# Delta-rule attention and two feed-forward layers: the inverses' write-out moved behind the next blocks' read, the read-out cut into 64-by-64 products

## The reference

```python
for t in range(S):                       # state: (B, H, 40, 40)
    y[:, :, t] = einsum('bhd,bhde->bhe', rt, state)
    Sa = einsum('bhde,bhe->bhd', state, at)
    state = state * wt[:, :, None, :] - einsum('bhd,bhe->bhde', Sa, bt)
    state = state + einsum('bhd,bhe->bhde', vt, kt)
x = y.transpose(0, 2, 1, 3).reshape(B * S, H * D)
h = x @ w_in;  solu = h * softmax(h);  x = layernorm(solu) * g_ln @ w_out
h = x @ w2_in; out = (max(h, 0) + alpha * min(h, 0)) @ w2_out
```

## Time and profile before

| | us |
|---|---|
| Time before, median of 3 runs | 1008.28 (1002.13 to 1009.63) |
| The profiled execution's own time | 1000.47 |
| Span of its trace | 998.7 |
| Mean granted TensorE clock | 0.966 |
| `solve_u` of step 0, 2, 20 starts at | 61.57, 97.22, 377.77 |
| Start of the last step (23) | 429.22 |

### The profile page before, as it was taken

How to read it: one execution, slowest core, us unless ns; L and a number is a source line. 1 busy time by engine, 2 the same in 40 slices (tenths; PEclk the granted TensorE clock), 3 DMA queues, 4 the chain that set the end, 5 groups by cost and what they waited for, 6 DMA issues and landing times.

```text
span 998.7 us, 31704 instructions
## 1 busy us (share of the span) xinstructions
PE 911.7 (91%) x13408; PEld 860.7 (86%) x13408; DVE 635.8 (64%) x1087; ACT 477.5 (48%) x1011; POOL 252.4 (25%) x452
## 2 busy tenths in 40 slices
PE   3379989998798987888999999999999999999998
PEld 2378888988797986777899999999999999999998
DVE  8957766776576754557756656565757565565644
ACT  3336655565454654436534435353535344443533
POOL 9577655775567621000000000000000000000000
PEclk9689989999999999998999999999999999999999
DMA  5635655557465552243010000000000000000000
GB/s 159 134 80 138 160 117 123 143 139 172 92 149 160 122 112 60 84 145 109 14 27 1 27 11 17 27 0 26 0 26 0 26 0 26 0 26 14 1 14 14
DMA packets 144095, 67.35 MB, mean 67 GB/s; under 512 B 118844, under 2 KB 129980, under 8 KB 143980
## 3 DMA queue, kind: packets, MB, share of 16 engines
q1 hardware_dynamic: 143980, 65.66, 26.5%
HBM read 45.98 MB, written 19.66 MB: 66 GB/s over the span
## 4 chain that ended last, share of the span: by engine, by line
PE 51%; POOL 15%; DMA 12%; DVE 8%; issue 6%; SPq 4%; ACT 3%; POOLq 0%; ACTq 0%; DVEq 0%
POOL s_x L831 6%; PE acc L1116 6%; POOL s_t L829 5%; PE acc L1117 5%; PE acc L1118 5%; DMA l_scr<-lb 5%; PE mid L1116 4%; PE mid L1117 4%; PE mid L1118 4%; PE bank L1116 3%; PE bank L1117 3%; PE bank L1118 3%; DMA s_in<-l_scr 3%; DMA d_scr<-s_x 3%; PE bank L1149 2%
## 5 line engine op out<-in xcount | busy, mean ns | idle before, releaser
L1382 POOL TENSOR_TENSOR stats<-stats 128x1 f32<-128x1 f32 x24 | 13.2, 549 | 552.3 <-DVE stats L1444 552.3
L1469 DVE SCALAR_TENSOR_TENSOR stage<-mid,slopes 128x512 f32<-128x512 f32 x96 | 66.3, 691 | 105.2 <-ACT slopes L1310 105.2
L1306 ACT ACTIVATE stage<-mid 128x512 f32<-128x512 f32 x96 | 57.1, 594 | 158.2 <-PE mid L1187 158.2
L1116 PE MATMUL acc<-wo_h,act_h 128*128 128x320 f32 x384 | 121.4, 316 | 6.7 <-DVE act_l L1396 5.9
L1117 PE MATMUL acc<-wo_h,act_l 128*128 128x320 f32 x384 | 118.4, 308 | 0.0
L1118 PE MATMUL acc<-wo_l,act_h 128*128 128x320 f32 x384 | 117.9, 307 | 0.0
L1116 PE MATMUL mid<-zT_h,w_h 128*128 128x256 f32 x384 | 108.0, 281 | 3.2 <-DVE zT_l L1396 3.2
L1117 PE MATMUL mid<-zT_h,w_l 128*128 128x256 f32 x384 | 107.6, 280 | 0.0
L1118 PE MATMUL mid<-zT_l,w_h 128*128 128x256 f32 x384 | 107.4, 280 | 0.0
L808 POOL TENSOR_TENSOR al<-al,prod 40x512 f32<-40x512 f32 x48 | 74.0, 1541 | 93.1 <-DMA al<-a_features_first 77.6
L1310 ACT ACTIVATE slopes<-stage,minus_alpha 128x256 f32<-128x256 f32 x192 | 87.3, 502 | 3.1
(11 more groups left out here) (163 smaller groups left out, 2401.1 us busy)
## 6 DMA issues: line engine op xcount, KB each, us to landing
wkb<-wkb_features_first SPq DMA_DIRECT2D x46, 242.5 KB
rvu<-rv_features_first SPq DMA_DIRECT2D x48, 160.0 KB
l_scr<-lb SPq DMA_DIRECT2D x24, 256.0 KB, 4.4
x_scr<-x SPq DMA_DIRECT2D x24, 256.0 KB, 4.6
al<-a_features_first SPq DMA_DIRECT2D x48, 80.0 KB
sv<-v_time_first SPq DMA_DIRECT2D x48, 80.0 KB, 3.5
out<-y_sb SPq DMA_DIRECT2D x11, 320.0 KB, 2.3
d_scr<-s_x SPq DMA_DIRECT2D x12, 256.0 KB, 2.1
```

The lines of the kernel that those rows point to most:

```text
L1116: pe.matmul(o, left[0], right[0], start=start, stop=False)
L1306: act.activation(neg[q % 2][:], mid[q % 2][:], ACT.Relu, scale=-1.0).then_inc(neg_ready, 1)
L1469: dve.scalar_tensor_tensor(out=act_f[q % 2][:], in0=mid[q % 2][:], scalar=0.0, in1=slope[q % 2][:], op0=ALU.max, op1=ALU.add).then_inc(act ...
```

## The change

On SP, `d_write` and `d_read` of a pair leave the odd step n-1 and go into the even step n, behind `l_read` of the next pair; `load_wkb`, `save_y` and `load_rv` stand between them now. On ACT, `spread_d` goes behind `take_state`. On PE, `read_out` makes for each head four products of one half's 40 rows by one slot, 64 columns each, on four quarters of the array; the halves have a bank each, the wait and the signal are one for the whole, and DVE masks half by half.

```diff
@@ sync, step(n)
             if n % 2 == 0 and n + 4 < NG:
                 l_read((n + 4) // 2)
+            inverses = n % 2 == 0 and 0 < n < NG - 2
+            if inverses:
+                d_write(n // 2 + 1)
             if n + 8 < NG:
                 load_wkb(n + 8)
             if n > 0:
                 save_y(n - 1)
             if n + 2 < NG:
                 load_rv(n + 2)
-            if n % 2 == 1 and n + 3 < NG:
-                d_write((n + 3) // 2)
+            if inverses:
+                d_read(n // 2 + 1)
             if n + 3 < NG:
                 load_v(n + 3)
-            if n % 2 == 1 and n + 3 < NG:
-                d_read((n + 3) // 2)
@@ tensor, read_out(m)
-            for piece in range(2):
-                wait(pe, q_ready, 2 * m - 1 + piece)
-                for h in range(piece * 4, piece * 4 + 4):
-                    for slot in range(2):
-                        ins = pe.matmul(pq[HR[slot], h * P:(h + 1) * P], vuT[m % 3][:, slot, h], r_bd[m % 3][:, :, h],
-                                        start=True, stop=True)
-                ins.then_inc(q_done, 1)
+            wait(pe, q_ready, 2 * m)
+            for h in range(NH):
+                for half, slot in [(0, 0), (1, 1), (0, 1), (1, 0)]:
+                    col = half * 512 + h * T
+                    ins = pe.matmul(pq[HR[slot], col:col + T], vuT[m % 3][ER[half], slot, h],
+                                    r_bd[m % 3][ER[half], half, h], start=True, stop=True)
+            ins.then_inc(q_done, 1)
@@ vector
-        def mask_q(m, piece):
+        def mask_q(m, half):
-            dve.wait_ge(q_done, 2 * m + 1 + piece)
+            dve.wait_ge(q_done, m + 1)
             wait(dve, y_done, m)
-            dve.tensor_tensor(q[:, piece * 4:piece * 4 + 4].rearrange("p n a t -> p (n a) t"),
-                              pq[:, piece * 512:piece * 512 + 512].rearrange("p (n t) -> p n t", t=T),
-                              repeated(later, slice(0, P), 8), ALU.mult).then_inc(q_ready, 1)
+            dve.tensor_tensor(q[:, :, half], heads(pq[:, half * 512:half * 512 + 512], NH, T),
+                              repeated(later, slice(0, P), NH), ALU.mult).then_inc(q_ready, 1)
@@ scalar, step(n)
-            if n % 2 == 0 and n + 2 < NG:
-                spread_d(n // 2 + 1)
             beside(act, n, "mid")
             if 0 < n < NG - 1:
                 take_state(n - 1)
+            if n % 2 == 0 and n + 2 < NG:
+                spread_d(n // 2 + 1)
             if n + 2 < NG:
```

## The result

The changed kernel takes 1060.42 us (median of 4 runs, 1058.76 to 1069.86) against 1007.69 us before: 1.055 times the time, 95% interval 1.048 to 1.063, slower by 53 us. The forecast was 1035 us with a range up to 1060. The sign and the place were right, the size was not. On the chip of e1 to e4, eight of the 19 runs of the kernel before count as slow; the means of all 19 and of the other 11 are 1006.0 and 1001.5 us, so a ratio there moves by half a per cent with the choice.

A forecast was written before the change was run, and what follows sets the result against it. In steps 2 to 19 GpSimd's inverses and SP's waits for them, not PE, were taken to set the pairs. +33.5 for nine pairs, -3.3 and -3.5 gave +27 us on the median 1008.28: 1035 us, range 1003 to 1060.

The forecast's parts named there:

- the 0.3 us for the transfers ahead of `d_read`: SP's queue, even step: estimate added to `d_read`'s 4.6 us landing for three bulk transfers ahead, landing at t+14.4.
- t+9.5: SP, even step: `d_read` leaves 9.5 us after the step's start t, behind `d_write` and the three bulk transfers.
- The bound: Even step, forecast 19.1 us: between 17.8 and 20.6 us, the upper with `d_read` at 5.3 us and one slow SP issue.
- Odd step: Steps after the even step's stall: 15.8 us, lengthened by PE's fallen clock, bounds 13.2 and 17.5.
- GpSimd: Inverse ready at t+27, SP asks at t+35+6; nearly all of SP's 79.8 us of waiting goes.
- Step 20: PE's 3.27 us idle behind ACT's wait for `d_write(11)` goes: -3.3 us, range 0 to -3.3.
- Read-out: PE's read-out in quarters falls from 1.88 to 1.0 us, worth -3.5 us in steps 1, 20, 21 and 22.
- The sum: Whole kernel: +33.5 us for nine pairs, -3.3 for step 20, -3.5 for the read-out, +26.7 us together.
- A: Rival: clock holds through the 5 us gaps, or the gap falls to 3 us; pair 32.3, total 1011 us; chance 0.17.
- B: Rival: inverse is in `dc` before ACT asks, pairs fall to 26.4 to 28.2 us, total about 966; chance 0.05.
- C: Rival: same chain, shorter than any row; even step 16.5, clock kept, pair 29.7, total 988 us; chance 0.06.
- D: Rival: the read-out's weight loads are serial, forecast plus 8, 1043 us; a third of the forecast's case.

The follow-up runs named there:

- e1: Changed kernel with read-out and masks as before, only the order on SP and ACT new: 1061.23 us, 1.055 times the kernel before.
- e4: Changed kernel with `d_write` and `d_read` moved between `load_a` and `l_read`: 1006.73 us, 1.006 times the kernel before.
- e3: Changed kernel with `d_read` directly behind `d_write`, the three bulk loads and saves behind it: 1034.13 us, 1.029 times the kernel before.
- e9: Changed kernel with `load_wkb` alone behind `d_read`, `save_y` and `load_rv` still ahead: 1046.45 us, 1.036 times the kernel before.
- e8: Changed kernel with `d_write` alone ahead of `l_read`, `d_read` still behind `load_rv`: 1056.35 us, 1.056 times the kernel before.
- e7: Changed kernel with 28 unread products on PE at the end of even steps 2 to 18: 1043.02 us, 1.039 times the kernel before.
- e5: Changed kernel with `d_write` ahead of the odd step's `l_write`, `d_read` right behind it, `spread_d` ahead of `take_state`: 986.96 us, 0.986 times the kernel before.
- e12: Changed kernel with `d_write`, `d_read` around `l_write`, the even step's `load_a` ahead of `d_write`, old read-out: 978.74 us, 0.969 times the kernel before.

## Why the prediction was wrong in size

- **The step that failed is the 0.3 us for the transfers ahead of `d_read`.** The sum let it land 4.9 us after its issue, 4.6 as before and 0.3 for the loads. It took 7.0 us in the mean of the nine, and 4.1 to 4.2 with nothing ahead (e3), so the loads cost 2.8 us, ten times the term.
- **Why it was so small.** The rule of the Trainium skill ("DMA: Bandwidth & Descriptors", queues, rings and completion order) that a DMA engine takes a ring's descriptors in order was weighed, allowed 1 us at most and left out of the sum, since the 3 us of issue seemed to cover 3 us of bytes. Each of the two loads was counted as one DMA where it is two: 658 KB for 1061. At the same 221 GB/s 1061 KB are 4.9 us, an estimate, and the first of them left only 2.1 to 3.0 us ahead of `d_read`; 1.9 to 2.8 us remain, where the seven steps with all of them show 3.3, so 0.5 us or more has no account. By that rule, with the bytes counted right, the even step of the forecast comes to 20.7 to 21.6 us; e3, e9 and the steps 16 to 20 agree with it.
- **The other link that was too short is SP's own issue.** `d_read` was to leave at t+9.5 and left at 10.4 in the mean: `l_read` went at 6.0 (5.6 said), and the issue of `d_write` behind it took 1.0 to 2.5 us instead of 0.43. In e8, where `l_read` isn't ahead of it, it took 0.4 in eight of nine steps. From the start of ACT's copies to `solve_u` 4.7 us were forecast, and step 12 shows 318.03 - 313.27 = 4.76. Together the even step is 22.1 us instead of 19.1: 2.1 us from the landing, 0.9 from the issue. Times nine this is 27 of the 28.6 us by which the steps 2 to 19 went past the forecast.
- **The bound.** The even step was bounded at 20.6 us by the slowest `d_read` of the earlier trace rows. In the steps 2 to 18 none of those had more than `load_v`'s two 80 KB ahead of it and behind `d_write`; a bound from rows in which the new neighbour is missing is none. That the pair, 38.1 us, is no longer than its upper bound is luck: that bound adds an odd step of 17.5 us to the even one of 20.6.
- **Odd step: right.** 15.8 said, 15.9 measured, and its reason holds: with the clock kept (e7) it is 13.6, the bound that was given was 13.2. The clock of the steps 2 to 19 was said to fall to 0.91 and fell to 0.87; PE's waits for `rhs` were 7.2 us in the mean of the nine and not 5 to 6.
- **GpSimd: right.** It finishes long before SP asks; SP doesn't wait for it at `d_write`.
- **Step 20:** 3.3 us were to go, 2.3 went. The wait for `d_write(11)` did go, and PE idled 3.80 us ahead of step 21's `solve_u` in its place, behind a late `dc` as in the other even steps.
- **Read-out:** 1.0 us, all four quarters at once, right (the 1.0 us that the forecast took for 32 records from the earlier trace rows is the busy time of the weight loads; PE's own record is 1.15). That it would be worth 3.5 us isn't shown: the changed kernel and e1, which differ in it alone, measure 1060.42 and 1061.23 us, ratios 1.055 and 1.055.
- **The sum.** The span grew by 60.5 us where 26.7 were forecast. Of the 33.8 us between them 28.6 are in the steps 2 to 19 and 1.0 in step 20; the rest is the read-out's 3.5, which did not show, and 0.7 elsewhere. The medians are 53 us apart and not 60, because the profiled execution of the kernel before was 7 us quicker than its median.
- **Rivals.** A (clock kept) falls by the 0.87, B (prefetch pays) by the chain in SP's order, C by e3, which with the landing at 4.1 us was still at 19.1, D by 0.98 us. The change's idea was sound: with the inverse DMAs around `l_write` the next blocks leave early and `l_read` no longer stands between the block write and the inverse (e5, 0.986; e12, 0.969).

## What to carry to other kernels

A queue in program order has two costs when an item is moved behind another: the wait of the item ahead, and the bytes of the items ahead, even where nothing waits for them. Before moving a small transfer that an engine waits for, add up the bytes that will stand ahead of it, DMA by DMA from the page and not load by load, and charge it with what their issue time does not cover. When a wait on one engine is taken away, look for the next fixed point that the chain is tied to: here it went from GpSimd's end, which adapts, to the end of the previous step, which comes once in every pair, and the idle gap costs again through the clock.

## What the runs showed that was not expected

- In the read-out in quarters four records of matmul, one on each quarter, start every 58 ns, the time in which two of `horner`'s do: 64 records in 0.98 us. The Trainium skill ("TensorEngine Tiling (Array Packing)", Key Properties) has it that different tiles can load weights and multiply in parallel, and the trace agrees. But with them came 10 to 25 us of pauses without a cause in the profile, against 5 to 9 with halves.
- The landing of one 256 KB transfer made of small pieces: 4.1 us with nothing ahead of it in the queue, 5.0 to 5.9 with 576 KB and 7.2 to 8.0 with 1061 KB in the changed kernel.
- PE kept busy with work for nobody, 6.6 us in each gap, made the kernel 17 us faster than the same kernel idle.
